# Attention and two MLPs on one core: the end of batch 0, with GpSimd making the high halves of the first two weight blocks

## The reference

```python
k_p = k.reshape(B, H, Sp, pool, D).mean(axis=3)       # B, H, S, D = 8, 8, 576, 64; pool = 8; Sp = 72
v_p = v.reshape(B, H, Sp, pool, D).mean(axis=3)
scores = scale * np.matmul(q, k_p.transpose(0, 1, 3, 2))
scores = scores - np.max(scores, axis=-1, keepdims=True)
attn = np.exp(scores)
attn = attn / (np.sum(attn, axis=-1, keepdims=True) + 1e-09)
x = np.matmul(attn, v_p)                              # then to [4608, 512]
h = np.maximum(x @ w_in, 0.0)                         # w_in [512, 2048], w_out [2048, 512]
x = h * h @ w_out
h = x @ w_in2
g = np.where(h >= 1, h, np.where(h <= -1, 0.0, (h + 1) ** 2 / 4.0))
out = g @ w_out2
```

## Time and profile before

| | |
|---|---|
| device time, 3 runs | 1772.68 us median, 1771.05 to 1774.06 |
| the profiled execution | 1771.15 us, its span 1769.4 us |
| PE busy | 1751.3 us (99% of the span) |
| DVE, ACT, POOL busy | 761.8, 553.7, 229.7 us |
| PE on the chain that ended last | 96% of the span |

### The profile page before, as it was taken

How to read it: one execution, slowest core, us unless ns; L and a number is a source line. 1 busy time by engine, 2 the same in 40 slices (tenths; PEclk the granted TensorE clock), 3 DMA queues, 4 the chain that set the end, 5 groups by cost and what they waited for, 6 DMA issues and landing times.

```text
span 1769.4 us, 22412 instructions
## 1 busy us (share of the span) xinstructions
PE 1751.3 (99%) x8371; PEld 1413.9 (80%) x8371; DVE 761.8 (43%) x1211; ACT 553.7 (31%) x970; POOL 229.7 (13%) x254
## 2 busy tenths in 40 slices
PE   8999999999999999999999999999999999999999
PEld 6777777777777777778888788888888888888887
DVE  6664434444444443433235434343434343434343
ACT  5453333333333333332234322222222222222222
POOL 6332313223131231310000000000000000000000
PEclk8999999999999999999999999999999999999999
DMA  6453324242331423213035202020201020201000
GB/s 153 126 153 122 85 71 120 65 124 81 104 99 59 130 74 118 84 61 107 1 116 170 95 1 72 1 71 0 71 0 71 0 71 0 71 0 71 0 24 24
DMA packets 117062, 126.86 MB, mean 72 GB/s; under 512 B 40192, under 2 KB 72448, under 8 KB 116992
## 3 DMA queue, kind: packets, MB, share of 16 engines
q1 hardware_dynamic: 116992, 125.86, 23.1%
HBM read 80.74 MB, written 45.09 MB: 71 GB/s over the span
## 4 chain that ended last, share of the span: by engine, by line
PE 96%; DVE 2%; ACT 1%; issue 0%; DMA 0%; POOL 0%; SPq 0%; ACTq 0%
PE ps_h L931 44%; PE ps_y L968 44%; PE ps_a L882 2%; PE ps_a L906 2%; PE ps_a L919 2%; PE ps_a L896 1%; DVE sq_f L726 1%; DMA first_kv<-in_v 0%; PE ps_h L941 0%; ACT act_f L569 0%; PE ps_y L863 0%; PE ps_y L852 0%; DVE probs L664 0%; DVE stat L662 0%; POOL first_kv L434 0%
## 5 line engine op out<-in xcount | busy, mean ns | idle before, releaser
L931 PE MATMUL ps_h<-xc,w_hi 128*128 128x512 f32 x2288 | 715.1, 394 | 0.0
L931 PEld LDWEIGHTS ps_h<-xc,w_hi 128*128 128x128 f32 x2288 | 423.0, 188 | 93.4 <-issue 9.2
L931 PE MATMUL ps_h<-xc,w_lo 128*128 128x512 f32 x1144 | 446.7, 390 | 0.0
L968 PE MATMUL ps_y<-w_hi,g_hl 128*128 128x512 f32 x1152 | 379.6, 391 | 3.1 <-DVE stage L750 2.2
L968 PE MATMUL ps_y<-g_hl,w_hi 128*128 128x512 f32 x1152 | 366.3, 399 | 1.5 <-DVE g_hl L730 1.5
L726 DVE TENSOR_TENSOR sq_f<-act_f 128x512 f32<-128x512 f32 x144 | 111.4, 774 | 414.0 <-ACT act_f L569 414.0
L968 PEld LDWEIGHTS ps_y<-w_hi,g_hl 128*128 128x128 f32 x1152 | 217.1, 188 | 49.0 <-DVE stage L750 2.6
L968 PEld LDWEIGHTS ps_y<-g_hl,w_hi 128*128 128x128 f32 x1152 | 209.7, 188 | 57.2 <-issue 15.3
L576 ACT ACTIVATE act_f<-act_f,half_bias 128x512 f32<-128x512 f32 x144 | 104.2, 724 | 480.2 <-DVE act_f L737 480.2
L931 PEld LDWEIGHTS ps_h<-xc,w_lo 128*128 128x128 f32 x1144 | 214.5, 188 | 46.4
L968 PE MATMUL ps_y<-g_hl,w_lo 128*128 128x512 f32 x576 | 225.7, 392 | 0.0
(11 more groups left out here) (81 smaller groups left out, 945.9 us busy)
## 6 DMA issues: line engine op xcount, KB each, us to landing
mlp_out_hl<-stage SPq DMA_DIRECT2D x36, 512.0 KB, 4.3
xc<-mlp_out_hl SPq DMA_DIRECT2D x36, 512.0 KB, 5.7
xc<-attn_out_hl SPq DMA_DIRECT2D x32, 512.0 KB, 3.9
attn_out_hl<-xo_hl SPq DMA_DIRECT2D x56, 288.0 KB, 2.3
out<-stage SPq DMA_DIRECT2D x36, 256.0 KB, 2.1
stage<-in_moe_w_in SPq DMA_DIRECT2D x32, 256.0 KB, 3.6
stage<-in_moe_w_out SPq DMA_DIRECT2D x32, 256.0 KB, 4.7
kv_raw<-in_k SPq DMA_DIRECT2D x28, 288.0 KB
```

The costliest lines, as they stand in the source:

```text
L931: mm = nc.tensor.matmul(ps_h[:, f % 2, :], left[:, f, kd * P:(kd + 1) * P], xc[:, buf, right, kd, :], start=(kd == 0 and n == 0), stop=(kd ...
L968: mm = nc.tensor.matmul(ps_y[:, m, :], left, right, start=(f == 0 and n == 0), stop=(f == NF - 1 and n == 2))
```

## The change

The change touches the first 60 us of the program, that is batch 0 and the first hidden and output blocks of chunk 0.

- Loads: k of head pair 0 is issued ahead of q. TensorE pools k (`first_pool_k`, now a function of its own) ahead of turning q, and ScalarE copies k ahead of q. The number of `keep_warm` matmuls goes up by 3 in three places.
- GpSimd's list: the scalings of a unit come between the adds of v, in place of behind both first blocks of them. GpSimd also makes `w_hi` of blocks 0 and 1 (`first_w_hi`), each in two halves of 512 columns, and `w_lo` in halves too. A new semaphore `w_first_hi` counts the halves.
- ScalarE no longer makes `w_hi` of blocks 0 to 2 between the units. Block 2 goes to the start of chunk 0, behind both calls of `hidden1`. VectorE's `w_lo` of block 2 goes to the same place.
- The factor 1/8 of the pooling moves from the sums' TENSOR_SCALAR into the copy to `p_t`; the eps is added by a TENSOR_TENSOR with a constant tile `eps_t`. TensorE turns the probabilities into PSUM with a step of 3 elements, so that ScalarE's copy reads and writes in one run of 576.
- TensorE's list at the end of batch 0 is another: first by blocks in `first_hidden`, and `hidden(At(0), 0, 2, 0)` stands ahead of the first output in place of behind it.

The diff (the declarations of `eps_t` and `w_first_hi` left out):

```diff
@@ -253,7 +255,7 @@
                 if 4 <= n < 6:
-                    sp.wait_ge(w_first, n - 3)
+                    sp.wait_ge(w_first, n - 1)
                 elif n >= 6:
@@ -358,8 +360,8 @@
 
+            first_load_k(0)
             first_load_q(0)
-            first_load_k(0)
             first_load_k(1)
@@ -414,7 +416,8 @@
             nc.gpsimd.memset(k_bd[:], 0.0).then_inc(zeroed, 1)
-            pool.wait_ge(zeroed, 4)
+            nc.gpsimd.memset(eps_t[:], EPS).then_inc(zeroed, 1)
+            pool.wait_ge(zeroed, 5)
             nc.gpsimd.affine_select(out=ident[:], in_=ident[:], compare_op=ALU.not_equal, fill=1.0, base=0,
@@ -439,9 +442,15 @@
 
-            def first_w_lo(n):
-                pool.wait_ge(w_hi_done, n + 1)
-                nc.gpsimd.tensor_tensor(w_lo[:, n, :], stage[:, n, :], w_hi[:, n, :].bitcast(F32),
+            def first_w_hi(n, half):
+                part = slice(half * DM, (half + 1) * DM)
+                pool.wait_ge(w_loaded[n], 2 * DMA)
+                nc.gpsimd.tensor_copy(w_hi[:, n, part], stage[:, n, part]).then_inc(w_first_hi, 1)
+
+            def first_w_lo(n, half):
+                part = slice(half * DM, (half + 1) * DM)
+                pool.wait_ge(w_first_hi, 2 * half + n + 1)
+                nc.gpsimd.tensor_tensor(w_lo[:, n, part], stage[:, n, part], w_hi[:, n, part].bitcast(F32),
                                         ALU.subtract).then_inc(w_first, 1)
@@ -470,24 +479,32 @@
 
-            for hp in range(2):
-                for i in range(3):
-                    first_add_v(hp, i)
+            for i in range(3):
+                first_add_v(0, i)
             first_scale(0)
+            first_add_v(1, 0)
             first_scale(1)
+            first_add_v(1, 1)
+            first_add_v(1, 2)
+            first_scale(2)
             first_add_v(2, 0)
-            first_scale(2)
+            first_scale(3)
             first_add_v(2, 1)
-            first_scale(3)
             first_add_v(2, 2)
+            first_scale(4)
             first_add_v(3, 0)
-            first_scale(4)
+            first_w_hi(0, 0)
+            first_scale(5)
             first_add_v(3, 1)
-            first_scale(5)
             first_add_v(3, 2)
+            first_w_hi(1, 0)
             first_scale(6)
-            first_w_lo(0)
-            first_w_lo(1)
+            first_w_lo(0, 0)
+            first_w_lo(1, 0)
+            first_w_hi(0, 1)
+            first_w_hi(1, 1)
+            first_w_lo(0, 1)
+            first_w_lo(1, 1)
             for s in range(SLOTS):
@@ -515,11 +532,14 @@
             def first_copy_q(u):
+                if u == 0:
+                    act.wait_ge(k_turned, 1)
+                    copy_k(first_q_bank(1))
                 act.wait_ge(q_turned, u + 1)
                 copy_q(first_q_bank(u))
-                if u % 2 == 0:
+                if u and u % 2 == 0:
                     act.wait_ge(k_turned, u // 2 + 1)
-                    copy_k(first_q_bank(u + 1))
+                    copy_k(first_q_bank(1))
 
@@ -528,8 +548,7 @@
                 act.wait_ge(probs_turned, u + 1)
-                nc.scalar.copy(p_t[:].rearrange("n a (p j) -> n a j p", j=NJ),
-                               ps_y[0:SP_, 0:2, 0:HALF].rearrange("n a (j p) -> n a j p", j=NJ)).then_inc(p_copied, 1)
+                nc.scalar.activation(p_t[:], ps_y[0:SP_, 0:2, 0:HALF], ACT.Copy, scale=1.0 / POOL).then_inc(p_copied, 1)
 
@@ -588,6 +607,8 @@
                 for f in range(NF):
+                    if layer == 1 and c.at(0) and f == 0:
+                        split_w(2)
                     if layer == 1 and c.at(0) and f + 3 < NF:
@@ -625,8 +646,6 @@
                     first_copy_q(u + 2)
-                if u >= 5:
-                    split_w(u - 5)
             first_x_hi(NU - 3)
@@ -649,7 +668,7 @@
             def split_w(n):
-                dve.wait_ge(w_hi_done, n + 1)
+                dve.wait_ge(w_hi_done, n - 1)
                 nc.vector.tensor_tensor(w_lo[:, n % NF, :], stage[:, n % 4, :], w_hi[:, n % NF, :].bitcast(F32),
@@ -693,8 +712,8 @@
                 dve.wait_ge(sum_done, u + 1)
-                nc.vector.tensor_scalar(stat[:, u % 2, 2, :], stat[:, u % 2, 1, :], EPS, float(POOL),
-                                        ALU.add, ALU.mult).then_inc(eps_done, 1)
+                nc.vector.tensor_tensor(stat[:, u % 2, 2, :], stat[:, u % 2, 1, :], eps_t[:],
+                                        ALU.add).then_inc(eps_done, 1)
                 dve.wait_ge(eps_done, u + 1)
@@ -783,14 +804,12 @@
                     first_sums(u - 1)
-                if u >= 3:
+                if 3 <= u < NU - 1:
                     first_x_lo(u - 3)
...
             last_scale()
-            first_x_lo(NU - 3)
-            first_x_lo(NU - 2)
-            split_w(2)
-            first_x_lo(NU - 1)
+            for u in range(NU - 4, NU):
+                first_x_lo(u)
             hidden1(At(0), 0)
@@ -821,14 +840,15 @@
                 mm.then_inc(q_turned, 1)
-                if u % 2 == 0:
-                    pe.wait_ge(k_first[u // 2], DMA)
-                    for e in range(POOL):
-                        for a in range(2):
-                            mm = nc.tensor.matmul(first_q_bank(u + 1)[a * D:(a + 1) * D, HALF:HALF + SP_],
-                                                  first_k[:, u // 2, a, e * D:(e + 1) * D], ident[0:SP_, 0:SP_],
-                                                  start=(e == 0), stop=(e == POOL - 1))
-                    mm.then_inc(k_turned, 1)
+
+            def first_pool_k(hp):
+                pe.wait_ge(k_first[hp], DMA)
+                for e in range(POOL):
+                    for a in range(2):
+                        mm = nc.tensor.matmul(first_q_bank(1)[a * D:(a + 1) * D, HALF:HALF + SP_],
+                                              first_k[:, hp, a, e * D:(e + 1) * D], ident[0:SP_, 0:SP_],
+                                              start=(e == 0), stop=(e == POOL - 1))
+                mm.then_inc(k_turned, 1)
 
@@ -849,7 +869,7 @@
                     for j in range(NJ):
-                        mm = nc.tensor.transpose(ps_y[0:SP_, a, j * QT:(j + 1) * QT],
+                        mm = nc.tensor.transpose(ps_y[0:SP_, a, 0:HALF].rearrange("n (p j) -> n j p", j=NJ)[:, j, :],
                                                  first_p[:, u % 3, (2 * j + a) * SP_:(2 * j + a + 1) * SP_],
@@ -933,25 +953,28 @@
 
+            def first_hidden(f, left, right, blocks, start=False, stop=False):
+                for kd in blocks:
+                    mm = nc.tensor.matmul(ps_h[:, f, :], left[:, f, kd * P:(kd + 1) * P], xc[:, 0, right, kd, :],
+                                          start=(start and kd == blocks[0]), stop=stop)
+                if stop:
+                    mm.then_inc(h_ready, 1)
+
             def first_hidden_hi(f, blocks):
-                pe.wait_ge(w_hi_done, f + 1)
-                for kd in blocks:
-                    pe.wait_ge(x_split, 2 * kd + 2)
-                    for right in range(2):
-                        nc.tensor.matmul(ps_h[:, f, :], w_hi[:, f, kd * P:(kd + 1) * P], xc[:, 0, right, kd, :],
-                                         start=(kd == 0 and right == 0), stop=False)
+                pe.wait_ge(w_first_hi, f + 1)
+                pe.wait_ge(x_split, 2 * blocks[-1] + 2)
+                first_hidden(f, w_hi, 0, blocks, start=(0 in blocks))
+                first_hidden(f, w_hi, 1, blocks)
 
...
                 pe.wait_ge(w_first, f + 1)
-                for kd in blocks:
-                    mm = nc.tensor.matmul(ps_h[:, f, :], w_lo[:, f, kd * P:(kd + 1) * P], xc[:, 0, 0, kd, :],
-                                          start=False, stop=(kd == KD - 1))
-                if KD - 1 in blocks:
-                    mm.then_inc(h_ready, 1)
+                first_hidden(f, w_lo, 0, blocks)
 
...
 
+                if c.at(0) and f < 2:
+                    pe.wait_ge(w_first, f + 3)
                 pe.wait_ge(g_ready, c.times(NF, f + 1))
@@ -978,7 +1001,9 @@
                     fixed = c.off if c.reg is None else None
-                    if f + 2 < NF:
+                    if fixed == 0 and f == 0:
+                        pass
+                    elif f + 2 < NF:
                         weights = 0 if fixed == 0 else NF if fixed == NC else None
@@ -990,37 +1015,48 @@
             pe.wait_ge(consts_ready, 1)
+            first_pool_k(0)
             first_turn_q(0)
-            keep_warm(2)
+            keep_warm(3)
             first_scores(0)
             first_turn_q(1)
-            keep_warm(1)
+            keep_warm(2)
             for u in range(NU - 1):
...
                     first_turn_q(u + 2)
+                if u % 2 == 0 and u + 2 < NU:
+                    first_pool_k(u // 2 + 1)
                 if u < 2:
-                    keep_warm(2)
+                    keep_warm(2 + u)
                 if u >= 2:
...
                     first_turn_p(u - 1)
```

(28 more changed lines are left out.)

## The result

The changed kernel takes 1776.85 us in the median of 11 runs (1774.46 to 1779.74), the kernel before 1770.65 in 11 runs beside it (1768.49 to 1774.06). The ratio is 1.0035, with an interval of 1.0025 to 1.0044: slower by 6 us, 0.35%. The forecast was 1773.8, so the time lies inside the range of 1768.5 to 1778.5, but the likeliest case (within 0.2%) did not come. The profiled execution took 1778.73 us with a span of 1776.9, 7.5 more than the span before.

The account below looks back on a forecast made before the run. PE was taken to bound the kernel, with 96% of the chain. Terms: -7.0 up to hidden block 0, +6.0 before hidden block 2, +0.8 copies, +2.5 clock, -0.4 behind, together +1.9; forecast 1773.8 us, range 1768.5 to 1778.5.

Parts of the forecast that it names:

- The start: Program start: GpSimd scales unit 0 sooner, turn 0 moves from 16.63 to 15.5; 1.2 us gained with k's copy hidden.
- The strided turn: Turning probabilities into PSUM: ScalarE's copy falls from 0.94 to 0.63 us, PE's strided write costs nothing.
- Rival 2: Strided turn is slow: doubled transposes add 0.6 us a unit, +5.4 in all, 1777.3; chance 0.14.
- The casts: GpSimd's 128x512 casts of weights in the tail of batch 0: taken as 0.8 us each, between 0.46 and 1.2.
- The tail: Last units of batch 0: product 6 waits till 35.3, hidden block 0 complete at 40.0 against 47.0, 7 us gained.
- What gives it back: Hidden block 2 waits for VectorE's low half, taking turns with GpSimd's adds, till 48.1; +6.0 us.
- The copies: Ahead of batch 1's first scores: ScalarE's copies of q and k, 0.40 and 0.45, no longer covered; +0.8 us.
- The stop behind it: PE's stop of 1.44 us at 65.3, after output 1 starts: 0.4 us gained, between 0 and 1.44.
- The clock: PE's clock falls during the stop before hidden block 2; half rate for 5.1 us loses 2.5, bounds 1.2 to 5.
- rival 3: Clock falls already in the tail: hidden block 0 at 42.3, almost no cost; 0.1 that it stays low, 1775.9.
- Sum at output 1: Start of output 1, 55.98 before: forecast at 58.3, 2.3 us later.
- slower: Whole kernel slower than the forecast's bound of +3.5 us, through rival 2 or rival 3; chance 0.24.

Follow-up runs that it names:

- the first experiment: The changed kernel with one wait more: GpSimd starts the weight blocks' last six instructions only after VectorE's last scaling; 1771.61 us, ratio 1.0001 to the kernel before.
- the version with waits: The changed kernel with GpSimd waiting for VectorE's last scaling, low half of weight block 2 and both differences, and weight block 2 split early; 1764.71 us, ratio 0.9969.
- the one with the sooner adds: The version with waits, but GpSimd's batch 1 adds wait for the first of VectorE's two differences, not the second; 1764.81 us, ratio 0.9957.

## Why the prediction was right or wrong

- **The start** (forecast: turn 0 at 15.5, scores of unit 7 at 27.9). The profile has 14.41 and 26.86. The mechanism held: the stop of 1.12 is gone. With the same code up to there, turn 0 was at 14.66 to 17.42 in the nine experiments on the changed kernel, so the 1.1 us beyond my term are no more than one execution differs from another.
- **The strided turn** (forecast: free on PE, 0.63 for the copy) was right: 0.69 and 0.65. The page "PSUM — Partial Sum Buffer" of the Trainium skill, Specifications, says that any non-contiguous access pattern slows matmuls significantly. These six transposes don't show it: they take 0.69 with the stride and 0.69 without it, and for this write the measurement decides. Rival 2 fell.
- **The casts** were shorter than I took (0.58 to 0.61 against 0.8); nothing hung on it.
- **The tail is the step that failed.** I wrote that "VectorE's last eps add no longer takes 3.95 us", and let its last scaling wait for one subtraction only. The add took 3.50 and the scaling 3.19. Product 6 started at 38.47 where I had 35.3 (3.2 us), and what stands from there to the relu took 9.4 at half the clock where I had 4.7. Hidden block 0 came at 47.90 and not at 40.0. The row of 3.95 was in my hands, and I even priced it in the next step. In this place I argued from the new instructions' size and not from what stood behind them on GpSimd: a longer run than before (31.44 to 37.49 against 33.50 to 38.18), still without an open wait. The page "SBUF — State Buffer" of the Trainium skill, Who interferes with whom, has the second to issue wait till the first instruction is finished. Here it waited through two to four (3.95, 3.50, 3.19, 4.66), and through one only where GpSimd waited too (0.48, 1.55).
- **What gives it back** (forecast: hidden block 2 at 48.1, 8.1 behind the relu's instant of 40.0). It came at 52.64, 4.7 behind 47.90: the squares now met no adds, as these were over at 42.45. That is my own figure without contention, 4.6. In the first experiment, with hidden block 0 at 39.88, it came at 47.01, so the step itself was sound and only mis-sized by 1.1.
- **The copies** that nothing covers: a stop of 0.88 ahead of batch 1's first scores, against 0.85. **The stop behind it**: 1.12 from 1.44, against a gain of 0.4.
- **The clock** (forecast: 2.5 lost behind the second stop). Hidden block 2 took 5.46 in place of 2.78, 2.7 lost. What I had not got was the first fall; rival 3 had it, but priced it as almost nothing, since it took hidden block 2's start as fixed at 48.3. With the first stop at 5.29 us that no longer held.
- **Sum at output 1:** 7.9 later up to the relu, 3.4 given back up to hidden block 2, 0.4 behind: 63.3 and not 58.3. The time exceeds the forecast by 3 us in the median and by 5.7 in the profiled execution, which lies 1.9 above its median. Against the kernel before it is +6.2 (1776.85 to 1770.65) where I had +1.9.

So the outcome is the one that I had called "slower", 0.24, by none of the rivals named for it. That the time still lies in the range is luck: the range was stretched upwards for the strided turn, which cost nothing, and the kernel before itself ran 2 us faster this time than in the runs that I started from. That the covered cost of the kernel before would be uncovered by making PE's list shorter ahead of it was the mechanism that I lacked.

## What to carry to other kernels

Look for every VectorE TENSOR_TENSOR with two operands in SBUF, and every TENSOR_SCALAR with one, that stands next to a run of GpSimd instructions with no open wait between them, and price it by the run's end, not by one instruction. A wait in GpSimd's code that is met when GpSimd gets there doesn't count; one at which it had to stand was worth 5 us here. A long stall that costs nothing is only covered: before you shorten the list that covers it, ask what the critical engine meets when it arrives there sooner. A long stop of PE costs its length and then the slow clock behind it: the two here stood still for 9.1 us (5.29 and 3.84), and with both put right the kernel was 12 us faster.

## What the runs showed of the hardware that I had not expected

- The 96x6 add took 0.16 to 0.69 us or 3.10 to 4.66, depending on what GpSimd had behind its current instruction. It never got in between two subtractions that follow one another without an open wait. But it got in between the two casts of the changed kernel, and the scaling did between the last subtraction and batch 1's first add (GpSimd's next row starts at 37.45, the scaling ends at 37.96), though no wait was open in either place. So an open wait is enough to let VectorE in (0.48, 1.55), but it isn't the only such place; why was not tried.
- Not every VectorE instruction with an operand in SBUF is held up. In the kernel before, a TENSOR_REDUCE of 96x432 took 0.60 us at 33.62 beside the first subtraction, the same as elsewhere, and a RECIPROCAL 0.19 at 38.24 beside an add of GpSimd's.
- PE's pace at the program's start is not the same from execution to execution. Pooling k (32 matmuls) in the changed kernel, then in the version with waits and the one with the sooner adds, whose start is the same code:

```profile
4.37 1.22 PE L848 MATMUL ps_a<-ident,first_kv 72*64 72x72 f32 x32
```

```profile
4.72 1.88 PE L850 MATMUL ps_a<-ident,first_kv 72*64 72x72 f32 x32
```

```profile
4.72 2.19 PE L850 MATMUL ps_a<-ident,first_kv 72*64 72x72 f32 x32
```

  The granted clock reads 1.00 from 2 to 12 us in all three, so these rows don't show whether the clock is the cause. A single profile can't judge a change of 1 us at this place.
